# An attention and two dense layers on one core: first layer in eight equal tiles of 288 tokens, two buffers of x, tiles that follow each other without a drain, and another order in the opening

## What is computed

```python
def _attn_ref(q, k, v):                     # 4 batches, 8 heads, 576 tokens, 64 wide
    factor = 4
    q_d = q.reshape(B, H, Sd, factor, D).mean(axis=3)      # k_d, v_d likewise: 144 groups
    out_up = np.repeat(sm_attn(q_d, k_d, v_d), factor, axis=2)
    mask = np.abs(pos[:, None] - pos[None, :]) < factor    # a band of 7 keys
    scores = np.where(mask, scale * np.matmul(q, k.transpose(0, 1, 3, 2)), -1000000000.0)
    ...
    return out_up + np.matmul(attn, v)

x = attn_out.transpose(0, 2, 1, 3).reshape(2304, 512)
h = x @ w_in;  r = np.maximum(h, 0.0);  x = (s * (r * r) + b) @ w_out      # 512 -> 2048 -> 512
h = x @ w2_in; return (h - np.tanh(h)) @ w2_out                            # 512 -> 2048 -> 512
```

## Time and profile before

| what | us |
|---|---|
| median of three runs (1023.90 to 1028.44) | 1024.55 |
| the profiled execution | 1032.04 |
| its span, first to last instruction | 1030.2 |
| PE busy (of the span) | 939.4 (91%) |
| DVE busy | 587.1 (57%) |
| ACT busy | 418.6 (41%) |
| POOL busy | 312.1 (30%) |

### The profile page before, as it was taken

How to read it: one execution, slowest core, us unless ns; L and a number is a source line. 1 busy time by engine, 2 the same in 40 slices (tenths; PEclk the granted TensorE clock), 3 DMA queues, 4 the chain that set the end, 5 groups by cost and what they waited for, 6 DMA issues and landing times.

```text
span 1030.2 us, 14837 instructions
## 1 busy us (share of the span) xinstructions
PE 939.4 (91%) x5552; PEld 870.7 (85%) x5552; DVE 587.1 (57%) x819; ACT 418.6 (41%) x1036; POOL 312.1 (30%) x307
## 2 busy tenths in 40 slices
PE   2549699899999898998999999999999999999997
PEld 1239689899999897998999998999999899998996
DVE  4992989789899989899700234232232232323322
ACT  2556255565456443543344554232222222322221
POOL 4577977647753632224223210000000000000000
PEclk9999899899899999999999998999999999999999
DMA  8941143433432322122012440020020100200101
GB/s 224 338 102 47 31 119 87 140 95 101 114 85 47 80 64 75 47 78 62 17 46 72 151 157 11 1 62 1 1 62 1 39 24 1 62 1 1 32 1 31
DMA packets 40200, 69.64 MB, mean 68 GB/s; under 512 B 5072, under 2 KB 20416, under 8 KB 40128
## 3 DMA queue, kind: packets, MB, share of 16 engines
q1 hardware_dynamic: 33216, 60.43, 20.8%
q10 hardware_dynamic: 6912, 8.26, 2.8%
HBM read 59.23 MB, written 9.44 MB: 67 GB/s over the span
## 4 chain that ended last, share of the span: by engine, by line
PE 71%; DVE 20%; DMA 3%; ACT 2%; issue 2%; POOL 1%; ACTq 1%; SPq 0%; DVEq 0%; POOLq 0%
PE acc L1233 20%; PE hid L1215 20%; PE acc L1196 14%; PE hid L1176 14%; DVE prod L818 5%; DVE prod L826 3%; DVE prod L831 3%; DVE sc L766 2%; DVE oloc L836 2%; DVE prod L759 2%; DMA x2T<-ystage 1%; DMA own<-in_q_dram 1%; PE pa L1119 1%; ACT ystage L1044 1%; DVE xfull L863 1%
## 5 line engine op out<-in xcount | busy, mean ns | idle before, releaser
L702 POOL TENSOR_TENSOR gl<-relu,gh 128x192 fp32r<-128x192 f32 (+1 forms) x128 | 130.7, 1022 | 249.2 <-ACT relu L1031 209.4
L1176 PE MATMUL hid<-xh,wah 128*128 128x192 f32 (+1 forms) x512 | 164.6, 322 | 14.2 <-ACT relu L1025 9.3
L1196 PE MATMUL acc<-gh,wbh 128*128 128x384 f32 (+2 forms) x512 | 164.0, 320 | 0.0
L1196 PE MATMUL acc<-gl,wbh 128*128 128x384 f32 (+2 forms) x512 | 160.4, 313 | 2.3 <-POOL gl L702 2.3
L888 DVE TENSOR_TENSOR gdif<-hid,tanh 128x384 f32<-128x384 f32 x96 | 53.4, 557 | 190.8 <-ACT tanh L1070 190.8
L1196 PE MATMUL acc<-gh,wbl 128*128 128x384 f32 (+2 forms) x512 | 160.0, 313 | 0.0
L1176 PE MATMUL hid<-xh,wal 128*128 128x192 f32 (+1 forms) x512 | 159.5, 312 | 0.0
L1176 PE MATMUL hid<-xl,wah 128*128 128x192 f32 (+1 forms) x512 | 157.4, 314 | 1.2 <-POOL xl L693 1.0
L1215 PE MATMUL hid<-x2h,wah 128*128 128x384 f32 x384 | 131.4, 342 | 4.2 <-DVE gdif L888 4.2
L1215 PE MATMUL hid<-x2h,wal 128*128 128x384 f32 x384 | 130.7, 340 | 0.0
L1215 PE MATMUL hid<-x2l,wah 128*128 128x384 f32 x384 | 130.6, 340 | 0.0
(11 more groups left out here) (90 smaller groups left out, 1585.4 us busy)
## 6 DMA issues: line engine op xcount, KB each, us to landing
wa_raw<-in_moe_w_in_dram SPq DMA_DIRECT2D x8, 1024.0 KB, 9.0
wb_raw<-in_moe_w_out_dram SPq DMA_DIRECT2D x8, 1024.0 KB, 9.1
kl<-in_k_dram SPq DMA_DIRECT2D x37, 192.0 KB
vl<-in_v_dram SPq DMA_DIRECT2D x37, 192.0 KB
x2raw<-x2T SPq DMA_DIRECT2D x6, 768.0 KB, 4.4
own<-in_q_dram SPq DMA_DIRECT2D x11, 384.0 KB
ql<-in_q_dram SPq DMA_DIRECT2D x44, 96.0 KB, 2.3
own<-in_v_dram SPq DMA_DIRECT2D x26, 144.0 KB
```

Of the source, the lines that this page charges most:

```text
L702: g.tensor_tensor(out=gl[:, turn % GRING1, 0:width(j)], in0=relu[:, f % 2, 0:width(j)], in1=gh[:, turn % GRING1, 0:width(j)].bitcast(F32), ...
L1176: one = pe.matmul(dst, w[:, d, cols], x[:, d, n], start=i == 0, stop=i == len(products) - 1)
L1196: one = pe.matmul(acc[:, d, n], w[:, f, cols], g[:, turn % GRING1, n], start=(f == 0 and p == 0), stop=(f == FT - 1 and p == 2))
```

## The change

- The first layer has `TILES1 = SUBS = 8` tiles of 288 tokens, and a sub of the attention is the same 288 tokens (NSUB = 2 a batch, 9 tokens a partition and head). Units are of five and four tokens, PE turns a sub in three parts, and `add_up` writes one to two tokens of all pairs in one instruction.
- x, xh and xl have two buffers (`XRING = 2`), and x lies in place of xl.
- `turns` orders the steps of a layer: the next tile's first hidden step comes ahead of the last two output steps of this tile, and no steps are missing at the boundary. The second layer uses it too, with two buffers of the split x2.
- `finish1` fills a `ystage` of four pieces; one `store1` on SP writes them.
- Opening: all loads are on SP, those of the first sub's q and k first; the fourteen stages of batch 0 have buffers of their own. POOL makes the q sums of batch 0, DVE the k sums; in batch 1 DVE makes q and k.
- The remainders of the first layer's weights for the first `FTURN = 6` steps are made on PE as raw x identity minus high x identity (`w1_rest`) and copied by ACT (`w1_place`); POOL makes the others, after the first part of sub 0 has been read.
- The score steps have four buffers (`SCORES = 4`); the sum's 1e-9 is added on ACT, and that of the band by an eighth column of `prob`.
- The planner's costs are changed, and PE's attention steps have a longer `lead`.

```diff
-NSUB = 3
+NSUB = 2
-UNIT = 3
-UNITS = [(h2, t0) for t0 in range(0, SUB, UNIT) for h2 in range(2)]
-PARTS = [(0, 2), (2, 4)]
+UNIT = 5
+UNITS = [(h2, t0, nt) for t0, nt in ((0, 5), (5, 4)) for h2 in range(2)]
+PARTS = [[(0, 4), (4, 4), (8, 1)], [(0, 3), (3, 4), (7, 2)]]
-TILE_SUBS = [1, 1, 1, 1, 2, 2, 2, 2]
-XRING = 4
+TILES1 = SUBS
+XRING = 2
+FTURN = 6
+SCORES = 4
+def vector_sums(b, n):
+    return (b == 0 and 3 <= n < 6) or (b == 1 and n < 6)
+def turns(tiles, lag):
+    steps = []
+    for t in range(tiles * FT):
+        j, f = divmod(t, FT)
+        steps.append(("hidden", t))
+        if j == 0 or f >= lag:
+            outputs = [t - lag] if t >= lag else []
+        elif f == lag - 1:
+            outputs = []
+        else:
+            outputs = [t - lag, t - lag + 1] if f == lag - 2 else [t - lag]
+        steps += [("output", one) for one in outputs]
+    return steps + [("output", t) for t in range(tiles * FT - lag, tiles * FT)]
-    dve = lambda n: 0.16 + 0.00104 * n
+    dve = lambda n: 0.17 + 0.00105 * n
+    add = lambda n: 0.32 + 0.00107 * n
+            if f < FTURN:
+                o.add("PE", 1.1, (2, f), ("w1_rest", f, half),
+                      [("w1_high", f, half)] + ([("w1_place", f - 1, half)] if f else []))
+                o.add("ACT", act(512), (2, f), ("w1_place", f, half), [("w1_rest", f, half)])
...
+            elif kind == "store1":
+                j, = key
+                sp.wait_ge(s_y, KT * (j + 1))
+                sp.dma_start(dram(x2T, j * NS, [[TOKENS, P], [P * TOKENS, KT], [1, NS]]), ystage[:, :, :]
+                             ).then_inc(s_stored, 16)
...
             elif kind == "x_low":
                 j, d = key
-                if j and d == 0:
-                    g.wait_ge(s_h, FT * j)
...
             elif kind == "add_up":
-                        ve.wait_ge(s_xl, KT * split_before(s))
+                        ve.wait_ge(s_h, FT * (s - XRING + 1))
...
             elif kind == "x_high":
-                    if j:
-                        sc.wait_ge(s_h, FT * j)
-                sc.activation(xh[:, d, 0:width(j)], xfull[:, d, xcols(j)], ACT.Copy).then_inc(s_xh, 1)
+                    if j >= XRING:
+                        sc.wait_ge(s_h, FT * (j - XRING + 1))
+                sc.activation(xh[:, j % XRING, d, :], xraw[:, j % XRING, d, :], ACT.Copy).then_inc(s_xh, 1)
...
             elif kind == "finish1":
+                if j:
+                    sc.wait_ge(s_stored, 16 * j)
                 for d in range(KT):
-                    sc.activation(ystage[:, slot, 0:width(j)], acc[:, d, 0:width(j)], ACT.Identity,
-                                  bias=bias[:, d:d + 1], scale=sb_s[:, 0:1]).then_inc(s_y, 1)
-                    sc.wait_ge(s_y, KT * j + d + 1)
-                    sc.dma_start(dram(x2T, FIRST[j] * NS + d * P * TOKENS, [[TOKENS, P], [1, width(j)]]),
-                                 ystage[:, slot, 0:width(j)]).then_inc(s_stored[slot], 16)
+                    sc.activation(ystage[:, d, :], acc[:, d, 0:NS], ACT.Identity, bias=bias[:, d:d + 1],
+                                  scale=sb_s[:, 0:1]).then_inc(s_y, 1)
...
+            elif kind == "w1_rest":
+                pe.matmul(hid[:, half, :], ident[:, :], half_of(f, half, wa_raw, wb_raw), start=True, stop=False)
+                pe.matmul(hid[:, half, :], minus[:, :], half_of(f, half, wah, wbh), start=False, stop=True
+                          ).then_inc(s_w1rest, 1)
...
             elif kind == "hidden1":
                 if j == 0:
-                    pe.wait_ge(s_w1low, 2 * f + 1)
+                    wait_low(pe, f, 0)
+                    if f == 0:
+                        pe.wait_ge(s_w1place, 2 * FTURN)
```

More of the change, by code:

```diff
@@ L218, in plan @@
[L218 to L219 removed]
+            o.add("SP", 0.6 * loads, (0, b, 2 * (s % NSUB) + (i == 2), i), (kind, s),
+                  [(user, s - 1, len(UNITS) - 1)] if s else [], kbytes=kbytes)
+        for a, (h2, t0, nt) in enumerate(UNITS):
+            o.add("DVE", add(nt * BAND * HD), (1, s, a), ("key_products", s, a),
                   [("load_queries", s), ("load_keys", s)], takes="prod")
[L221 removed]
@@ L227, in plan @@
[L227 to L231, removed]
+        o.add("DVE", 1.0, (0, s, 5), ("band_norm", s), [("band_exp", s)])
+        for a, (h2, t0, nt) in enumerate(UNITS):
+            after = [("band_norm", s), ("load_values", s)]
+            if s and a == 0:
+                after.append(("columns", s - 1, NPART - 1))
+            o.add("DVE", add(nt * BAND * HD), (1, s, 6 + a), ("value_products", s, a), after, takes="prod")
+            o.add("DVE", add(3 * nt * HD) + add(2 * nt * HD) + add(nt * HD), (1, s, 6 + a), ("value_sums", s, a),
@@ L232, in plan @@
                   [("value_products", s, a)], gives="prod")
-        for part, (t0, nt) in enumerate(PARTS):
-            after = [("value_sums", s, 1 if part == 0 else 3), ("place_up", b, NPAIR - 1)]
+        for part, (t0, nt) in enumerate(PARTS[s % NSUB]):
+            after = [("value_sums", s, 1 if t0 + nt <= UNIT else 3), ("place_up", b, NPAIR - 1)]
             if s >= XRING:
[L236 to L239, removed]
+                after += [("x_low", s - XRING, KT - 1), ("hidden1", s - XRING, FT - 1)]
+            o.add("PE", 0.11 * nt, (0, b, s), ("columns", s, part), after, 1.0 if s else 0.0, fills=True)
+            o.add("DVE", sum(0.28 + 0.14 * n for t, n in RUNS[s % NSUB][part]), (0, s), ("add_up", s, part),
+                  [("columns", s, part)], empties=("columns", s, part))
@@ L242, in plan @@
     chain = None
     for j in range(TILES1):
-        n = TILE_SUBS[j] * NS
-        after = [("add_up", s, 1) for s in range(FIRST[j], FIRST[j] + TILE_SUBS[j])]
-        after += [("hidden1", j - 1, FT - 1)] if j else []
+        after = [("add_up", j, NPART - 1)] + ([("hidden1", j - XRING, FT - 1)] if j >= XRING else [])
         for d in range(KT):
-            o.add("ACT", act(n), (0,), ("x_high", j, d), after)
-            o.add("POOL", pool(n), (0,), ("x_low", j, d), [("x_high", j, d)])
@@ L454, in build @@
     last_unit = len(UNITS) - 1
-    added, count = {}, 0
-    for step in o.order["DVE"]:
-        if step[0] == "add_up":
-            count += PARTS[step[2]][1] - 1
-            added[step[1:]] = count
     def dram(t, offset, pattern):
@@ L992, in scalar_program @@
                 if b and hp == 0:
-                    for part in range(len(PARTS)):
+                    for part in range(NPART):
                         ra, ma = bank("columns", b * NSUB - 1, part)
```

487 lines of the change are left out of this document (250 added, 237 removed).

## The result

The changed kernel takes **965.87 us** (median of four runs, 964.59 to 967.24); the kernel before took 1026.49 on the same chip. The ratio is 0.9408, 95% interval 0.9374 to 0.9443: 61 us faster. The forecast was 956 us, range 922 to 990, faster by over 0.5% with a chance of 0.95. Sign and range hold; the time is 10 us above the forecast, of which 2.4 lie in the span (963.4 against 961) and the rest in the scaling: the profiled execution took 965.22 us and lies at the median, not above it as that of before.

A forecast was written before the change was run, and what follows sets the result against it. PE was taken as the bound from 70.3 us on. The span of 1030.2 + 4 - 38 - 9 - 10 - 10 - 6 = 961 us, plus 1.8 and times 0.9927, gave 956 us, range 922 to 990.

The forecast's parts named there:

- Opening, +4: Before the first layer: earlier ql and kl loads against longer sub 0 and added pairs; PE begins near 74 us, +4 us.
- Width, -38: First layer: 3072 matmuls of 288 columns at 0.1302 us take 400.0 instead of 438.2 us, -38 us (-45 to 0).
- The bound above (0.1427): First layer, worst case: straight line between 192 and 384 columns, 0.1427 us a matmul, 438.4 us and no gain.
- the rival of 0.121: First layer, form of better than summed: a 288-column matmul takes 0.121 us, 28 us less, 928 us; better case chance 0.17.
- the very edge that the prediction set: First layer: twelve matmuls in 1.54 to 1.6 us; over 1.65 the width term is wrong.
- Waits of PE in the first layer, -19 with -9 for relu, -10 for oloc and 0 for POOL: First layer: relu's 9.3 us go, half of oloc's 19.9 stay, POOL's 5.3 stay (0 to 12).
- Clock, -10: First layer: with fewer waits, 10 of the 19 us lost to the low clock come back, -10 us (-19 to 0).
- Second layer, -6: Second layer: without ACT's four stores, PE's 4.18 us wait and the low-clock stretch behind it go, -6 us (-8 to 0).
- DVE as the bound: First layer: POOL stretches DVE's units, a sub takes 59 us, level with PE; at 62 us a sub, 977; chance 0.15.
- The better case: Faster matmuls (928 us), or oloc waits and low clock gone with the opening 4 us earlier (929); chance 0.17.
- the late opening: Opening: PE begins at 85 us, giving 967 us; chance 0.11.
- the wait for prob: First layer: DVE's 18.11 us wait for ACT's prob becomes the rule; at 21 us lost a sub, 1041 us; chance 0.03.

The follow-up runs named there:

- the narrow run: Changed kernel with first-layer matmuls cut to 256 columns (inner hidden products) and 224 (output steps 1 to 14); measured 0.120 and 0.111 us a matmul.
- the version with four steps on PE: Against the changed kernel: PE makes four steps' weight remainders instead of six, POOL's no longer wait for sub 0, g_low precedes later weight remainders; 960.11 us.
- the last version: Against the version with four steps on PE: six steps' remainders on PE, made between tile 0's layer steps in the attention's two banks; 962.92 us.

## Why the prediction was right, and where it was off

- **Opening, +4: measured +7.1.** Its parts hold: kl at 13.15 instead of 20.85, sub 0 longer, PE beginning on the last placement, and the order at SP is worth 10 us when undone. x(0) came at 72.1, 3 us past the 66 to 69; from there PE needed 5.3 us where 6 were reckoned. The transposes of sub 0 stood behind pairs in PE's order, most behind one and the last behind two more, and DVE waited 2.4 and 0.5 us for them ahead of x. A pair took 1.1 us at the full clock and 2.3 at the lower, as reckoned.
- **Width, -38: measured -29.6** (438.2 less 3072 x 0.133). This is the term that was mis-sized. I scaled the 384 row by its columns; the narrow run shows that 13 ns of a matmul do not scale, so 288 lie at 0.133, not 0.1302. The bound above (0.1427) and the rival of 0.121 were both wrong, the first because 192 lies on a floor, the second because nothing of that floor reaches 288. Twelve matmuls in 1.58 to 1.65 us stand at the very edge that the prediction set. No run undoes the width alone.
- **Waits of PE in the first layer, -19 with -9 for relu, -10 for oloc and 0 for POOL: measured -16.7.** All its waits were 37.4 us and are 20.7. The sum is right, the parts are not: oloc -19.7, relu -9.3, POOL +7.1 (6.3 to 13.4), k sums and x on DVE +6.2, ACT otherwise -1.0. I took half of oloc for lasting because I read it as DVE being late; the run with the old costs shows that the written order made a part of it, 5.8 us. The rest of why oloc's waits went is open. Those for relu went as forecast, but the order of the steps alone did not take them away: with the old order 0.7 us came back, with one buffer as well 1.3. What else changed there, above all the stores and their waits that left ACT's list, no run puts back, so that part of the term is argued and not shown. And I left POOL's waits as they were, with up to 12 allowed, where a look at POOL's list of tile 0 shows 20 remainders and 16 gl on an engine that is busy 67.7 of 71.7 us.
- **Clock, -10.** 0.97 became 0.98 over 478 us: (2 x 0.03 x 539 - 2 x 0.02 x 478)/2 = 6.6 us, and tile 0 no longer starts slowly, about 3: as taken. Two digits for so long a stretch are coarse: by windows of 50 us some 37 us lay at the lower level before and 17 after, 10 us, and with the slow start 13.
- **Second layer, -6: measured -13.** 4.18 us of wait and a low-clock stretch behind it went, as reckoned. PE also began it 2 us sooner after the last output step, and its 384-column matmuls run at 0.1736 instead of 0.1765 us, 3.3 us for 1152. These two I did not foresee; the alignment explains 1.1 us of the last, and its rest is open.
- Together the measured terms give 7.1 - 29.6 - 16.7 - 10 - 13 = -62 of the 66.8, or -65 with 13 for the clock; the other 2 to 5 us are not assigned. The sum came close by luck in part: the width brought 8 us less than taken, the second layer 7 more.
- **Rivals.** DVE as the bound came true in one place, tile 0: sub 1 took 71.7 us, for the reason that the rival named, POOL beside two-input instructions, and the run without POOL's remainders gives 15 us back, POOL's own time included. From sub 2 on a sub takes 51.4 us, as forecast, and PE is the bound. The better case did not come; nor did the late opening or the wait for prob (8.3 us in all, longest 3.1).

## What to carry to other kernels

A wait bears the name of whoever comes last; take its slack away and the next engine's name stands there, so count what is queued on every engine at that place before writing a wait down as gone. When an edit moves work between engines, look at the one stage in which both of them are full: here it was tile 0, where POOL's spare work was not spare, since it slowed DVE. And a gain ahead of a stage counts only as far as the next hand-over: PE's earlier start brought 1 us, because the next tile waited for DVE.

## What the hardware showed that was not expected

- A matmul with 192 or 224 columns follows the last after 0.111 us, one with 256, 288 or 384 after its columns at 2.4 GHz and 13 ns (0.120, 0.133, 0.1735).
- POOL's subtraction of 512 elements took 1.8 us beside DVE's products and 1.27 to 1.29 where DVE did little (69 to 72 us of the version with four steps on PE, shown above); its memset of 512 took 0.525, and DVE's value products then ran at 2.49 us, what the first product of the opening took.
- One product of DVE of 2.49 us took 6.42 beside a chain of POOL's subtractions, in the last version (DVE, then POOL):

```profile
141.85 6.42 DVE L791 TENSOR_TENSOR prod<-ql,kl 128x2240 f32<-128x2240 f32 x1
```
```profile
142.82 3.10 POOL L732 TENSOR_TENSOR xl<-xraw,xh 128x288 fp32r<-128x288 f32 x4
145.87 3.05 POOL L741 TENSOR_TENSOR gl<-relu,gh 128x288 fp32r<-128x288 f32 x1
```
